# Weight splits, a sixth opening pass and the start of the MLP units in a fused attention and two-layer kernel

## What is computed

```python
B, H, S, D = (4, 8, 576, 64)                      # float32
scores = (q @ k.T) / sqrt(D), masked above the diagonal
a = exp(scores - scores.max(-1)); a /= a.sum(-1) + 1e-09
local = a @ v
q_p = where(q > 0, q, exp(q) - 1) + 1
mem_out = (q_p @ M_prev) / (q_p @ z_prev + 1e-06)
g = sigmoid(beta)                                 # per head
attn = g * mem_out + (1 - g) * local              # (2304 tokens, 512)
h = attn @ w_in                                   # 512 -> 2048
y = where(h >= 1, h, where(h <= -1, 0, (h + 1) ** 2 / 4)) @ w_out
h2 = y @ w_in2
out = maximum(0.01 * h2, h2) @ w_out2             # (2304, 512)
```

## Time and profile before

| | value |
|---|---|
| median of 3 runs | 1052.85 us (1051.18 to 1053.05) |
| profiled execution | 1051.7 us |
| its span | 1049.8 us |
| PE busy | 1020.2 us, 97% |
| ACT, POOL, DVE busy | 535.1, 432.9, 413.1 us |
| PE's share of the chain that ended last | 87% |
| DMA moved | 66.43 MB |

### The profile page before, as it was taken

The page is one execution under the profiler, slowest core; times in us unless marked ns, Lnnn a source line. Parts: engine busy times, 40 slices in busy tenths (PEclk is TensorE's granted clock), DMA queues, the critical chain, the costliest instruction groups (busy, mean ns, idle before and its releaser), DMA issues.

```text
span 1049.8 us, 18275 instructions
## 1 busy us (share of the span) xinstructions
PE 1020.2 (97%) x7008; PEld 920.2 (88%) x7008; DVE 413.1 (39%) x1077; ACT 535.1 (51%) x1172; POOL 432.9 (41%) x405
## 2 busy tenths in 40 slices
PE   6779999999999999999999999999999999999997
PEld 4569899999999999999999999888888888888896
DVE  5755555655555554555531237222111221212111
ACT  6656777776767767677753357322222322322221
POOL 1655755556454554644632248422222222222221
PEclk8889999999999999999999999999999999999999
DMA  6555222223222322322211046100100100000010
GB/s 193 141 138 144 55 78 55 67 81 72 79 60 66 87 63 59 89 56 68 67 38 42 21 161 202 40 21 1 61 21 1 61 21 1 32 29 1 1 41 21
DMA packets 88600, 66.43 MB, mean 63 GB/s; under 512 B 53825, under 2 KB 78017, under 8 KB 88513
## 3 DMA queue, kind: packets, MB, share of 16 engines
q1 hardware_dynamic: 87360, 61.07, 21.5%
q10 hardware_dynamic: 1152, 4.19, 1.2%
HBM read 54.53 MB, written 10.63 MB: 62 GB/s over the span
## 4 chain that ended last, share of the span: by engine, by line
PE 87%; issue 4%; POOL 4%; ACT 2%; DMA 2%; SPq 1%; DVE 1%; POOLq 0%; ACTq 0%; DVEq 0%
PE Hp L592 12%; PE Hp L594 12%; PE Hp L593 12%; PE Yp L614 7%; PE Yp L615 6%; PE Yp L616 6%; PE At L620 6%; PE At L622 6%; PE At L621 6%; PE At L541 4%; PE At L516 4%; PE At L465 3%; PE At L501 2%; DMA kraw<-kk 1%; POOL Gl L1144 1%
## 5 line engine op out<-in xcount | busy, mean ns | idle before, releaser
L1144 POOL TENSOR_TENSOR Gl<-Gl_raw,Gh 128x512 fp32r<-128x512 f32 x144 | 192.9, 1339 | 419.3 <-ACT Gh L817 418.9
L592 PE MATMUL Hp<-Xh,WAh 128*128 128x256 f32 (+1 forms) x704 | 218.5, 310 | 5.5 <-DVE Xl L995 5.5
L594 PE MATMUL Hp<-Xh,WAl 128*128 128x256 f32 (+1 forms) x704 | 213.1, 303 | 0.0
L593 PE MATMUL Hp<-Xl,WAh 128*128 128x256 f32 (+1 forms) x704 | 213.1, 303 | 0.0
L614 PE MATMUL Yp<-Gh,WBh 128*128 128x256 f32 x576 | 169.9, 295 | 0.5 <-POOL Gl L1144 0.5
L1011 DVE TENSOR_TENSOR Gl_raw<-Hp,Gl_raw 128x512 f32<-128x512 f32 x72 | 49.8, 692 | 296.8 <-ACT Gl_raw L809 296.8
L615 PE MATMUL Yp<-Gl,WBh 128*128 128x256 f32 x576 | 162.6, 282 | 0.0
L616 PE MATMUL Yp<-Gh,WBl 128*128 128x256 f32 x576 | 162.5, 282 | 0.0
L809 ACT ACTIVATE Gl_raw<-Hp 128x512 f32<-128x512 f32 x72 | 43.1, 598 | 229.6 <-PE Hp L594 229.6
L592 PEld LDWEIGHTS Hp<-Xh,WAh 128*128 128x128 f32 x704 | 134.5, 191 | 15.8 <-DVE Xl L995 7.0
L593 PEld LDWEIGHTS Hp<-Xl,WAh 128*128 128x128 f32 x704 | 134.8, 191 | 5.0
(11 more groups left out here) (143 smaller groups left out, 1957.4 us busy)
## 6 DMA issues: line engine op xcount, KB each, us to landing
WAl_raw<-w_in SPq DMA_DIRECT2D x12, 512.0 KB, 4.8
WBl_raw<-w_out SPq DMA_DIRECT2D x12, 512.0 KB, 4.0
Vs_raw<-vv SPq DMA_DIRECT2D x16, 320.0 KB, 3.3
yT_scratch<-xraw SPq DMA_DIRECT2D x9, 512.0 KB, 3.7
kraw<-kk SPq DMA_DIRECT2D x16, 288.0 KB, 3.9
prob<-yT_scratch SPq DMA_DIRECT2D x9, 512.0 KB, 4.4
bc<-rn_scratch SPq DMA_DIRECT2D x32, 128.0 KB, 2.9
out<-prob SPq DMA_DIRECT2D x8, 512.0 KB, 3.3
```

The costliest lines, as they stand in the source:

```text
L592: pe.matmul(h, WAh[:, f, j, :], xh, start=(j == 0), stop=False)
L593: pe.matmul(h, WAh[:, f, j, :], xl, start=False, stop=False)
L594: last = pe.matmul(h, WAl[:, f, j, :], xh, start=False, stop=(j == DT - 1))
L1144: gp.tensor_tensor(Gl[:, U % 2, :], act[:, U % 2, :], Gh[:, U % 2, :].bitcast(F32), ALU.subtract).then_inc(g_lo, 1)
```

## The change

It has four parts. (1) Of the first layer's weights only unit 0 (in pass 1) and unit 1 (ACT in pass 4, DVE and POOL in pass 5) are split in the opening passes; tiles 4 to 15 are split one every second tick from tick 49 to 71, in slots 6 to 8. ACT's loads of weight units move to the ends of passes 1, 2, 4 and 5, and in `split_unit` it makes `WAh` ahead of `WBh`. (2) Slot 5 becomes a sixth opening pass, and `G0` is 50, so the first `hidden` stands at ticks 46 and 47, behind the whole of slot 5 on PE. (3) In the opening passes SP loads q and k two slots ahead, sends `cut_norms` first, and issues `spread_factors` ahead of `store_tail`; ACT and DVE get another order too (DVE: `phi` minimum ahead of the probabilities, factors ahead of `split_slot`). (4) In slots from 6 on `split_slot` moves from k = 1 to k = 3 on ACT and DVE.

```diff
@@ -93,19 +93,21 @@
-G0 = 46
+G0 = 50
 G_END = G0 + 64 * CHUNKS + 2
 PLAIN = 8
-OPENING = 5
+OPENING = 6
 OTHER_BANKS = 6
-WEIGHTS_AT = {(5, 5): 8, (5, 7): 9, (6, 5): 10, (6, 7): 11, (7, 5): 12, (7, 7): 13, (8, 1): 14, (8, 5): 15}
-
-LOAD_WEIGHTS_AT = {(5, 1): 4, (5, 7): 5, (6, 7): 6, (7, 5): 7}
+UNITS_SPLIT = {1: 0, 4: 1}
+WEIGHTS_AT = {((48 + 2 * i + 1) // 8, (48 + 2 * i + 1) % 8): 4 + i for i in range(12)}
+
+UNITS_LOADED = {1: 1, 2: 2, 4: 3, 5: 4}
+LOAD_WEIGHTS_AT = {(6, 1): 5, (6, 5): 6, (7, 1): 7}
 FIRST_UNIT = [UNITS * c for c in range(CHUNKS + 1)] + [UNITS * (CHUNKS + 2 * d) for d in range(1, 5)] + [2 * UNITS * CHUNKS]
@@ -363,7 +365,7 @@
             def slot(n, k):
                 front, back, last = stage(n)
-                if k == 0 and front is not None and front + 1 < SLOTS:
+                if k == 0 and front is not None and OPENING + 2 <= front + 1 < SLOTS:
                     load_qk(front + 1)
...
@@ -384,15 +386,15 @@
             def opening(n):
                 front, back, last = stage(n)
-                load_qk(front + 1)
+                cut_norms(front)
                 if back is not None:
                     send_sums(back)
-                cut_norms(front)
+                load_qk(front + 2)
                 load_mz(front + 1)
+                if back is not None:
+                    spread_factors(back)
                 if last is not None:
                     store_tail(last)
-                if back is not None:
-                    spread_factors(back)
                 load_v(front)
...
@@ -433,6 +435,7 @@
...
             load_mz(0)
+            load_qk(1)
             sp.dma_start(gates[:, 0, :], beta.partition_broadcast(P)).then_inc(beta_in, 16)
...
@@ -715,7 +718,7 @@
...
                     exps(front, 0)
-                if k == 1 and last is not None:
+                if k == 3 and last is not None:
                     split_slot(last)
...
@@ -744,19 +747,23 @@
             def opening(n):
                 front, back, last = stage(n)
-                if n > 0:
-                    split_unit(n - 1)
+                if n == 1:
+                    split_unit(UNITS_SPLIT[n])
                 memory_out(front)
...
                 exps(front, 0)
+                if n == OPENING - 1:
+                    split_slot(last)
                 phi_exponent(front + 1)
-                if last is not None:
+                if last is not None and n < OPENING - 1:
                     split_slot(last)
                 exps(front, 1)
-                if n < OPENING - 2:
-                    load_unit(n + 1)
+                if n == 4:
+                    split_unit(UNITS_SPLIT[n])
+                if n in UNITS_LOADED:
+                    load_unit(UNITS_LOADED[n])
             def load_unit(u):
@@ -765,10 +772,10 @@
             def split_unit(u):
                 f = slice(2 * u, 2 * u + 2)
+                sc.wait_ge(wa_in[0][u], 16)
+                sc.activation(WAh[:, f, :, :].rearrange("p a j m -> p (a j m)"), WAraw[:, f, :, :].rearrange("p a j m -> p (a j m)"), ACT.Copy).then_inc(wa_hi, 2)
                 sc.wait_ge(wb_in[0][u], 16)
                 sc.activation(WBh[:, f, :].rearrange("p a m -> p (a m)"), WBraw[:, f, :].rearrange("p a m -> p (a m)"), ACT.Copy).then_inc(wb_hi, 2)
-                sc.wait_ge(wa_in[0][u], 16)
-                sc.activation(WAh[:, f, :, :].rearrange("p a j m -> p (a j m)"), WAraw[:, f, :, :].rearrange("p a j m -> p (a j m)"), ACT.Copy).then_inc(wa_hi, 2)
             def split_weights(s, f):
...
@@ -929,10 +936,10 @@
...
                     row_max(front, 1)
-                if k == 1 and last is not None:
-                    split_slot(last)
                 if k == 1 and coming is not None:
                     least_q(coming)
+                if k == 3 and last is not None:
+                    split_slot(last)
                 if k == 4 and back is not None and back < PLAIN:
...
@@ -952,17 +959,21 @@
...
                     lay_gates()
+                if n == 1:
+                    split_unit(UNITS_SPLIT[n])
+                least_q(front + 1)
                 if back is not None:
                     plain_weights(back)
-                least_q(front + 1)
+                if n == OPENING - 1:
+                    split_slot(last)
                 phi_sum(front + 1)
-                if last is not None:
-                    split_slot(last)
-                factors(front)
                 if back is not None:
                     plain_sum(back)
-                if n > 0:
-                    split_unit(n - 1)
+                factors(front)
+                if last is not None and n < OPENING - 1:
+                    split_slot(last)
+                if n == 5:
+                    split_unit(UNITS_SPLIT[4])
             def lay_gates():
...
@@ -1101,7 +1112,7 @@
...
                     if n == OPENING:
-                        gp.wait_ge(wa_lo, 2 * n - 2)
+                        gp.wait_ge(wa_lo, 4)
                         scale_memory(last)
...
@@ -1121,12 +1132,17 @@
             def opening(n):
                 front, back, last = stage(n)
+                if n == 1:
+                    split_unit(UNITS_SPLIT[n])
                 if last is not None:
-                    gp.wait_ge(wa_lo, 2 * n - 2)
+                    if last == 0:
+                        gp.wait_ge(wa_lo, 2)
+                    else:
+                        gp.wait_ge(x_done, last)
                     scale_memory(last)
                     finish(last)
-                if n > 0:
-                    split_unit(n - 1)
+                if n == 5:
+                    split_unit(UNITS_SPLIT[4])
             def split_unit(u):
```

## The result

The changed kernel takes 1055.82 us, the median of 9 runs (1055.5 for the eight without the one named below), against 1051.64 for the kernel before in 9 runs on the same chip: a ratio of 1.0031 [1.002, 1.0041]. I had forecast 1046.3, range 1043.2 to 1050.5, with a chance of 0.05 for slower. The profiled run here took 1053.7 us.

A forecast was written before the change was run, and what follows sets the result against it. PE's own work was taken as the bound. The first output 4.4 us earlier plus 2.1 us of work done ahead made 6.5, with slots 6 to 8 net zero: 1052.85 - 6.5 = 1046.3 us, range 1043.2 to 1050.5.

The forecast's parts named there:

- Pass 1: Opening pass 1: memory matrix lands 0.8 us earlier (0.8 later to 1.5 earlier), absorbed in pass 2, so no gain.
- Rival B: Opening stays bound by loads, passes 2 to 4 waiting for values and factors: gain 3.2 us, time 1049.6, chance 0.20.
- Pass 2, `Xl` off the path: Opening pass 2: the 2.1 us of `Xl` leave the path; next memory product 1.7 us earlier, 33.87 to 32.2.
- Pass 3, the spread: Opening pass 3: spread ahead of the tail's store breaks the 8.3 us series; PE's 7.7 us remain, ending at 39.9.
- Pass 4: Opening pass 4: rows of slot 2 done at 45.4, then 3.1 us of short steps; next memory product at 48.5, against 53.54.
- Pass 5: Sixth opening pass: rows of slot 3 ready at 53.1, `Xl` slowed to 2.1 us by POOL's split, hidden starts at 55.5.
- Hidden, 3.5 predicted: First hidden product: 3.5 us, against 3.1 at full clock, ending at 59.0.
- The new wait before the first output: First output product: PE waits 1.6 us for `Gl`, once; output starts at 67.2, against 71.57.
- Slots 6 to 8, net zero: Slots 6 to 8: 12 tiles split instead of 8, two new `Gl` waits against old ones gone; net zero, +1.1 to -3.
- Rival C: POOL becomes the bound in slots 6 to 8: 9 us of waits at six outputs, time 1055.3, chance 0.07.
- The chances: Whole kernel against the one before: 0.88 faster, 0.07 the same, 0.05 slower.

The follow-up runs named there:

- experiment 1: The changed kernel with SP loading the memory matrix ahead of norms, sums, q and k in the opening passes: 1048.29 us, ratio 0.9968 to the kernel before.
- experiment 2: The changed kernel with ACT's loads of weight units 1 to 4 moved to the ends of passes 0, 3, 4 and 5: 1050.91 us, ratio 0.9998.
- experiment 3: The changed kernel with SP loading the memory matrix ahead of q and k but still behind norms and sums: 1048.96 us, ratio 0.9974.
- experiment 4: The changed kernel with ACT holding each load of a weight unit until the next memory matrix has landed: 1050.16 us, ratio 0.9979.
- experiment 5: The kernel before with SP loading q and k two slots ahead, just before the memory matrix, in the opening passes: 1058.89 us, ratio 1.0068.
- experiment 8: experiment 1 with one load of weights fewer in the opening passes: 1046.7 us, ratio 0.9958 to the kernel before.
- experiment 10: experiment 8 plus the wait of experiment 4, with POOL holding its split of unit 1 until `Xl` is made: 1046.62 us, ratio 0.9957.

## Why the prediction was wrong

**Pass 1, the step that failed.** "SP issues two loads, about 1.0 us, ahead of the memory matrix, but 1 MB of weights no longer travels beside it ... It is absorbed in pass 2." I priced the two loads at the time of their issue, one microsecond, and only for the matrix that is read at the start of pass 1. For that one the sum was right: 14.08 less 0.8 is 13.3, measured 13.40. But I never asked when the matrices of slots 2 and 3 would land. The weights of units 1 and 2 are still loaded at the ends of passes 1 and 2, and the matrix travels beside them behind 320 KB: 2.68 and 3.49 us of waits that the sum puts at nothing. They are 6.2 us together, more than the 4.2 of the stretch, because PE's wait for the values in pass 2, 2.62 us before, is gone behind them; in experiment 1, where the matrix is in time, it is back with 2.25. Experiments 1 to 4 take these two waits away (0.4 us at most is left), and experiment 5 puts them into the kernel before. Rival B had q and k in it, but as a danger to values and factors, and it still ended at 1049.6.

**Pass 2, `Xl` off the path: right, then covered.** `Xl` took 0.42 us in passes 2 to 4. Timeline of DVE, passes 4 and 5:

```profile
52.64 0.42 DVE L1006 TENSOR_TENSOR Xl<-xt,Xh 128x256 fp32r<-128x256 f32 x1
...
60.59 2.11 DVE L1006 TENSOR_TENSOR Xl<-PTl_raw,Xh 128x256 fp32r<-128x256 f32 x1 [2.76 <-ACT Xh L794]
```

With the matrix in time slot 3's product stands at 32.34 in experiment 1 (predicted 32.2). Half of that is luck: pass 2 takes 11.02 us there, 0.75 less than before and not the 1.7 of the sum, and the rest comes from slot 2's product, which is at 21.32 and not at 22.10.

**Pass 3, the spread: right in size with the matrix in time.** 7.7 predicted; 8.44 with the change, 7.56 in experiment 1 (39.90 less 32.34), 7.94 in experiment 8, and 11.14 without the edit. Experiment 10 has 12.19 with the edit and the matrix in time, with 2.60 us of it a wait for the values, so 7.7 is what the pass can take and not what it always takes. That no weights are loaded in pass 3 was right too; the ones issued at 30.00, in pass 2, did their harm before it began.

**Pass 4: right.** 8.6 predicted, 8.26 measured.

**Pass 5: mechanism right, one term missed.** The spread was issued where the sum had it, 5.3 us after 44.81:

```profile
50.13 1.10 SPq L351 DMA_DIRECT2D PTl_raw<-rn_scratch  x2
```

Landing and the way to POOL took 6.3 us and not 4.0. ACT's next unit of weights left at 50.43, 0.3 us behind it. That this is the cause shows in experiments 1 and 8, which differ by these loads: with weights issued 0.1 us behind it the spread of this pass took 6.6 us to POOL's start (44.73 to 51.32), and without them 4.2 (44.74 to 48.96). The late landing is 2.3 of the 2.7 us. POOL's first step on the rows of slot 3, and its split of unit 1:

```profile
56.44 1.79 POOL L1100 TENSOR_TENSOR PTl_raw<-mem,PTl_raw 64x320 f32<-64x320 f32 x2 [6.24 <-issue]
...
60.06 2.35 POOL L1150 TENSOR_TENSOR WAl<-WAl_raw,WAh 128x1024 fp32r<-128x1024 f32 x1
```

`Xl` met that split at 60.59 and took 2.11 us, as predicted (2.1). In these rows the rule that the Trainium skill gives (SBUF — State Buffer, Who interferes with whom) holds with DVE as the loser: 0.42 without POOL beside it, 2.11 with it. The opposite case, POOL as the loser, is there too. The first `Gl` is issued at 73.89, while DVE's split of a tile (issued at 73.11, 1.36 us long) is still running:

```profile
73.89 1.72 POOL L1160 TENSOR_TENSOR Gl<-Gl_raw,Gh 128x512 fp32r<-128x512 f32 x1
```

The `Gl` at 110.57, with no such split beside its start, takes 1.29. The first output waits 0.35 us for `Gl`, less than these 0.43.

**Hidden, 3.5 predicted: 4.55** (62.75 to the scores at 67.30). PE came into it with the clock at 1.00, after 2.06 us without work. The clock then fell to the lower level (1.2 GHz), with 16 of the 24 products started at it. Window of that part, the granted clock third from the end:

```profile
63.44:66.84 3.40, 3.40 (x18) 3.40 (x17) 1.70 (x5) 0.00 (x0) 1.52 (x2) 0.50 1.05 334
```

Its products follow each other by 0.21 us, and by 0.12 at full clock, so the lower level costs 1.8 times the time and not twice, but it lasted for longer than I took. The extra 1.05 us are nearly all of the 1.2 us of the last stretch.

**The new wait before the first output: right in size, wrong in place.** 1.6 predicted for `Gl`. Measured: 0.35 for `Gl` and 1.15 at the turn (69.95). The trace names no releaser for the latter; DVE's row maxima of slot 6, the first half of which ends at 69.84, are what this place waits for in the code (`max_done`).

**Slots 6 to 8, net zero: right.** From the first output to the end 976.2 us pass, and 976.1 to 976.3 in experiments 1, 4 and 8; with the 2.1 of work done ahead added, this is the 978.2 of before. Rival C, the only one that ended slower, did not happen: PE waits 0.4 us for `Gl` there (0.35 at the first output), and 0.7 later, in the second layer, as before. It was slower for another reason.

**The chances.** 0.05 for slower rested on POOL alone. Two loads were moved ahead in SP's queue, and for none of those behind them did I compare issue plus landing with the start of the product that reads it. The kernel before would have shown the margin. Its memory product of slot 1 waited 1.14 us for the matrix already, and the matrix issued in pass 1 (18.59) landed 2.0 us later, 1.5 us ahead of the product at 22.10: one microsecond of issue and a slower landing use that up.

**Open.** Runs of one and the same version spread by 2 to 8 us (experiment 2: 1048.1 to 1055.6, experiment 4: 1044.2 to 1051.5), where the kernel before spreads by up to 5. That loads land in another order from run to run would explain it. Near to it comes this: the values of pass 2 were issued at 29.48 us in experiment 8 and at 29.52 in experiment 10, and landed 6.2 and 7.3 us later; but these are two kernels, and no pair of traces of one kernel shows it.

## What to carry to other kernels

A load that is brought forward is paid by whatever stands behind it in its queue, and by how much depends on what another queue issues just then: for each load passed, take its own issue time, its own landing and the start of its reader, in every pass and not in one. Edits that gain can be hidden by one late load of 64 KB; when a change loses, look for the single wait that rose before undoing the parts. And test a part in the kernel where it can act: the spread was worth nothing alone and 3.8 us once the rest was right.

## What I had not expected of the hardware

A load of 64 KB took 5.9 us to land (median of two) behind 320 KB on its own queue and beside 1 MB on another, and 2.3 us in the kernel before. With only one of the two in its way it landed in 2.1 to 3.7 us, and PE hardly waited (1.0 us in all in experiment 4, none in experiment 3).

PE's idle time fell with the change, 29.6 to 27.5 us, while the span rose by 2.1: its busy time rose by 4.2 for the same products. In the opening the same product with the values takes 3.95 us or 2.38 (the row at 58.30), so the sum of idle time, by which I meant to judge the change, is no measure of what was lost there. The starts of the passes are.
